# Eight pairs of weights at eight places modulo 512 bytes, and five block bodies that read their columns in five orders

## The reference

```python
# batch 2, sequence 6080, d_model 256, d_ff 2048
sig = 1.0 / (1.0 + np.exp(-f_logit))
f = lower_bound + (1.0 - lower_bound) * sig
i = 1.0 - f
for t in range(S):
    h = f[:, t] * h + i[:, t] * x[:, t]
    y[:, t] = h
...
h = y.reshape(B * S, D) @ w_in                   # 12160 x 256 by 256 x 2048
g = np.where(h > 0.0, h, np.exp(np.minimum(h, 0.0)) - 1.0)
return g @ w_out                                 # 12160 x 2048 by 2048 x 256
```

## Time and profile before

| | |
|---|---|
| median of 2 runs | 963.42 us (961.59 and 965.25) |
| the profiled execution | 962.05 us |
| its span, first to last instruction | 960.2 us |
| TensorE busy | 954.3 us (99%), 4362 matmuls |
| weight loads busy | 815.4 us (85%) |
| ACT, DVE, POOL busy | 790.1, 722.3, 628.8 us |
| granted TensorE clock | 1.000 on average |

### The profile page before, as it was taken

The page is one execution under the profiler, slowest core; times in us unless marked ns, Lnnn a source line. Parts: engine busy times, 40 slices in busy tenths (PEclk is TensorE's granted clock), DMA queues, the critical chain, the costliest instruction groups (busy, mean ns, idle before and its releaser), DMA issues.

```text
span 960.2 us, 15016 instructions
## 1 busy us (share of the span) xinstructions
PE 954.3 (99%) x4362; PEld 815.4 (85%) x4362; DVE 722.3 (75%) x916; ACT 790.1 (82%) x1424; POOL 628.8 (65%) x477
## 2 busy tenths in 40 slices
PE   9999999999999999999999999999999999999998
PEld 6999888888888888888888888888888888888887
DVE  6998876976886796697688679679768867966444
ACT  7989888878888888888888888888888788887775
POOL 2578796576667668557656755856775765676544
PEclk9999999999999999999999999999999999999999
DMA  7212012002101201100210210120021021001001
GB/s 273 68 33 95 0 34 66 34 1 78 55 1 55 77 1 44 55 33 1 75 55 0 66 66 0 45 66 20 23 65 44 0 76 55 0 0 46 1 1 45
DMA packets 23078, 42.02 MB, mean 44 GB/s; under 512 B 2560, under 2 KB 4096, under 8 KB 23040
## 3 DMA queue, kind: packets, MB, share of 16 engines
q1 hardware_dynamic: 22752, 41.10, 13.2%
q10 hardware_dynamic: 288, 0.46, 0.1%
HBM read 29.10 MB, written 12.45 MB: 43 GB/s over the span
## 4 chain that ended last, share of the span: by engine, by line
PE 96%; ACT 2%; DVE 1%; issue 1%; POOL 0%; ACTq 0%; POOLq 0%
PE acc L896 17%; PE acc L898 17%; PE acc L897 17%; PE h L868 14%; PE h L866 14%; PE h L867 14%; ACT e L472 1%; PE h L1010 1%; PE h L1002 1%; PE h L1004 1%; PE h L1003 1%; ACT e L466 1%; DVE x L628 0%; PE h L968 0%; ACT w_out_hi L505 0%
## 5 line engine op out<-in xcount | busy, mean ns | idle before, releaser
L336 POOL TENSOR_TENSOR g_lo<-e,g_hi 128x512 fp32r<-128x512 f32 (+1 forms) x384 | 516.4, 1355 | 325.5 <-ACT g_hi L480 324.0
L466 ACT ACTIVATE e<-h 128x512 f32<-128x512 f32 (+1 forms) x379 | 224.8, 593 | 124.6 <-PE h L868 90.3
L719 DVE SCALAR_TENSOR_TENSOR e<-e,h 128x512 f32<-128x512 f32 (+1 forms) x379 | 256.8, 678 | 70.2 <-ACT e L472 69.1
L896 PE MATMUL acc<-g_hi,w_out_hi 128*128 128x512 f32 (+1 forms) x768 | 291.1, 379 | 0.4 <-DVE w_out_lo L690 0.4
L898 PE MATMUL acc<-g_hi,w_out_lo 128*128 128x512 f32 (+1 forms) x768 | 291.0, 379 | 0.0
L897 PE MATMUL acc<-g_lo,w_out_hi 128*128 128x512 f32 (+1 forms) x768 | 290.9, 379 | 0.0
L472 ACT ACTIVATE e<-e 128x512 f32<-128x512 f32 (+1 forms) x384 | 241.3, 628 | 9.7 <-issue 1.2
L480 ACT CAST g_hi<-e 128x512 fp32r<-128x512 f32 (+1 forms) x384 | 232.1, 604 | 19.3 <-DVE e L719 19.3
L866 PE MATMUL h<-a_hi,w_in_hi 128*128 128x512 f32 x616 | 234.7, 381 | 0.0
L868 PE MATMUL h<-a_hi,w_in_lo 128*128 128x512 f32 x616 | 234.7, 381 | 0.0
L867 PE MATMUL h<-a_lo,w_in_hi 128*128 128x512 f32 x616 | 234.7, 381 | 0.0
(11 more groups left out here) (77 smaller groups left out, 556.0 us busy)
## 6 DMA issues: line engine op xcount, KB each, us to landing
opening<-forget_logit SPq DMA_DIRECT2D x44, 256.0 KB, 2.7
x<-value SPq DMA_DIRECT2D x44, 256.0 KB, 2.7
out<-out_sb SPq DMA_DIRECT2D x44, 256.0 KB, 2.0
w_in_raw<-w_in SPq DMA_DIRECT2D x8, 256.0 KB, 5.4
w_out_raw<-w_out SPq DMA_DIRECT2D x8, 256.0 KB, 6.5
out<-out_sb SPq DMA_DIRECT2D x4, 224.0 KB, 1.9
x<-value SPq DMA_DIRECT2D x3, 224.0 KB, 6.1
opening<-forget_logit SPq DMA_DIRECT2D x2, 224.0 KB, 6.3
```

Source lines behind the costliest of these rows:

```text
L336: nc.gpsimd.tensor_tensor(g_lo[:, t % RING, 0:w], e[:, t % TILES, 0:w], g_hi[:, t % RING, 0:w].bitcast(F32), ALU.subtract).then_inc(g_lo_r ...
L466: nc.scalar.activation(e[:, i, 0:w], bank_of(j, t)[:, 0:w], ACT.Relu, scale=-1.0).then_inc(r_ready, 1)
L719: nc.vector.scalar_tensor_tensor(e[:, t % TILES, 0:w], e[:, t % TILES, 0:w], -1.0, bank_of(j, t)[:, 0:w], ALU.add, ALU.max).then_inc(g_rea ...
L896: nc.tensor.matmul(bank, hi, g_h, start=opens, stop=False)
```

## The change

Two things are changed, and no instruction is added, removed or moved on any engine. Each matmul keeps its place, its weights and its number of columns.

The weights: each pair's row in the four weight tensors is 4 floats (16 bytes, `STEP = 1`) longer. Pair q of `w_in_lo` then lies at q x 16 bytes modulo 512: at 0, 16, 32 to 112. The eight rows of a tensor add 128 bytes to what lies behind it, so that pair q of `w_out_lo` is at 128 + 16 q, of `w_in_hi` at 256 + 16 q and of `w_out_hi` at 384 + 16 q. Modulo 128 bytes (32 columns, the length of a leap in the old order) all four are at 16 q. `out_sb` and the plain `lo` weights of pairs 0 to 3 that block 0 uses (`w_plain_lo`) move to 256 modulo 512. The moving operands stay at multiples of 512: the tensors behind the weights move by 512 bytes in all. `carry`, `slope` and `offset` move into the padding that stood before `opening`.

The orders: `in_order` takes a style (kind, number of groups, columns in a run, direction), and each body gets its own:

| blocks | style | how TensorE steps through 512 columns |
|---|---|---|
| 0 | (T, 4, 8, 0) | as before |
| 1 | (T, 1, 512, 0) | one after the other |
| 2 | (T, 2, 4, 0) | runs of 4, the next one 8 further, 64 times; two groups |
| 3, 5, 7, 9 | (T, 4, 8, 0) | as before |
| 4, 6, 8, 10 | (T, 4, 4, 0) | runs of 4, the next one 16 further, 32 times; four groups |
| 11 | (T, 4, 8, 1) | as before, but the four groups last to first |

```diff
+STEP = 1
...
-LINE = 8
-APART = 4
+T, N = range(2)
+FIRST_STYLE = (T, 4, 8, 0)
+STYLES = (((T, 1, 512, 0),) * 4, ((T, 2, 4, 0),) * 4, ((T, 4, 8, 0),) * 4, ((T, 4, 4, 0),) * 4, ((T, 4, 8, 1),) * 4)
...
-def in_order(columns):
-
-    return columns.rearrange("p (b a c) -> p a b c", a=APART, c=LINE)
+def in_order(columns, style):
+    if style is None:
+        return columns
+    kind, groups, run, down = style
+    if kind == T:
+        steps = columns.rearrange("p (b a c) -> p a b c", a=groups, c=run)
+    elif groups == 1:
+        steps = columns.rearrange("p (o b c) -> p o b c", o=1, c=run)
+    else:
+        steps = columns.rearrange("p (b a c) -> p b a c", a=groups, c=run)
+    if down % 2:
+        steps = steps[:, ::-1]
+    if down // 2 % 2:
+        steps = steps[:, :, ::-1]
+    return steps[:, :, :, ::-1] if down // 4 else steps
...
+        in_row, out_row = in_cols + 4 * STEP, out_cols + 4 * STEP
+
+        def by_product(room):
+            return room[:, :, 0:in_cols].rearrange("p q (k c) -> p q k c", k=PRODUCTS)
...
-        w_in_raw = nc.alloc_sbuf_tensor_at("w_in_raw", [P, PAIRS, PRODUCTS, P], F32, offset=weights_at)
-        w_in_lo = nc.alloc_sbuf_tensor_at("w_in_lo", [P, PAIRS, PRODUCTS, P], F32R, offset=weights_at)
-        w_out_at = weights_at + 4 * PAIRS * in_cols
...
+        w_in_raw = by_product(nc.alloc_sbuf_tensor_at("w_in_raw", [P, PAIRS, in_row], F32, offset=weights_at))
+        w_in_lo = by_product(nc.alloc_sbuf_tensor_at("w_in_lo", [P, PAIRS, in_row], F32R, offset=weights_at))
+        w_out_at = weights_at + 4 * PAIRS * in_row
...
-        w_in_hi = sb("w_in_hi", [P, PAIRS, PRODUCTS, P], F32R)
-        w_out_hi = sb("w_out_hi", [P, PAIRS, 2, D], F32R)
+        w_in_hi = by_product(sb("w_in_hi", [P, PAIRS, in_row], F32R))
+        w_out_hi = by_unit(sb("w_out_hi", [P, PAIRS, out_row], F32R))
...
-        sb("room_of_edge", [P, P - EDGE])
+        edge = sb("edge", [P, P - EDGE])
...
-        carry = sb("carry", [P, BATCH, HALVES, 1])
-        slope = sb("slope", [P, HALVES])
-        offset = sb("offset", [P, HALVES])
+        carry = edge[:, 0:BATCH * HALVES].rearrange("p (b i o) -> p b i o", b=BATCH, o=1)
+        slope = edge[:, 4:4 + HALVES]
+        offset = edge[:, 6:6 + HALVES]
...
-            whole(1, 1)
-            whole(2, 0)
+            whole(1, 1, STYLES[0], FIRST_STYLE)
+            whole(2, 0, STYLES[1], STYLES[0][-1])
             with nc.Fori(1, (BLOCKS - 2) // 2, engines=(mybir.EngineType.PE,),
                          hint_back_edge=True) as i:
-                whole(2 * i + 1, 1)
-                whole(2 * i + 2, 0)
+                whole(2 * i + 1, 1, STYLES[2], STYLES[3][-1])
+                whole(2 * i + 2, 0, STYLES[3], STYLES[2][-1])
             j = BLOCKS - 1
-            whole(j, 1)
+            whole(j, 1, STYLES[4], STYLES[3][-1])
```

More of the change, by code:

```diff
@@ L859, in _, with product @@
         def _(pe):
-            def product(j, par, q, k, bank, start=False):
+            def product(j, par, q, k, bank, style, start=False):
                 w = width(j)
@@ L868, in product, with second @@
                 return nc.tensor.matmul(into, lo, a_h, start=False, stop=True, skip_group_check=True)
-            def second(j, t, half):
+            def second(j, t, half, style):
                 w = width(j)
@@ L902, in second, with whole @@
                     done.then_inc(acc_half, 1)
-            def whole(j, par):
+            def whole(j, par, styles, before):
                 def m(q, back, i, half):
@@ L908, in m @@
                     if at >= 0:
-                        second(j, TILES * at + i, half)
+                        second(j, TILES * at + i, half, styles[q // 2])
                     else:
-                        second(j - 1, TILES * (PAIRS + at) + i, half)
+                        second(j - 1, TILES * (PAIRS + at) + i, half, before)
                 for q in range(PAIRS):
@@ L922, in whole @@
                         pe.wait_ge(g_ready, TILES * (n - 2) + C21 + 1)
-                    product(j, par, q, P1, trunk(q), start=True).then_inc(p1_done, 1)
+                    product(j, par, q, P1, trunk(q), styles[q // 2], start=True).then_inc(p1_done, 1)
                     if q == 0:
@@ L926, in whole @@
                     pe.wait_ge(g_ready, TILES * (n - 1) + C12 + 1)
-                    product(j, par, q, P5, h[:, 2], start=True).then_inc(p5_done, 1)
+                    product(j, par, q, P5, h[:, 2], styles[q // 2], start=True).then_inc(p5_done, 1)
                     m(q, 2, C21, 0)
@@ L967, in first_products @@
                         pe.wait_ge(w_plain_hi_ready, unit // 2 + 1)
[L968 to L969 removed]
+                        nc.tensor.matmul(in_order(first_bank(unit), FIRST_STYLE), plain_weights(unit, half)[0],
+                                         in_order(pieces[half][0], FIRST_STYLE), start=half == 0, stop=False)
                 for unit in range(OPEN):
                     w = TILE if unit < WIDE else SHORT
[L972 removed]
+                    bank = in_order(first_bank(unit)[:, 0:w], FIRST_STYLE)
                     if unit == 0:
                         pe.wait_ge(a_lo_ready[P1], 1)
[L975 removed]
+                    nc.tensor.matmul(bank, plain_weights(unit, 0)[0], in_order(pieces[0][1][:, 0:w], FIRST_STYLE),
                                      start=False, stop=False)
@@ L978, in first_products @@
                     for half in range(HALVES):
-                        nc.tensor.matmul(bank, plain_weights(unit, half)[1], in_order(pieces[half][0][:, 0:w]),
+                        nc.tensor.matmul(bank, plain_weights(unit, half)[1], in_order(pieces[half][0][:, 0:w], FIRST_STYLE),
                                          start=False, stop=False)
@@ L988, in first_product @@
                 b, unit = FIRST_TILES[t]
-                bank = in_order(first_bank(t)[:, 0:SHORT])
+                bank = in_order(first_bank(t)[:, 0:SHORT], FIRST_STYLE)
                 pe.wait_ge(w_plain_lo_ready[unit // 2], 1)
@@ L996, in first_product @@
                     hi, lo = plain_weights(unit, half)
-                    a_h, a_l = [in_order(part[:, 0:SHORT]) for part in a_parts(0, PLACE[b][half])]
+                    a_h, a_l = [in_order(part[:, 0:SHORT], FIRST_STYLE) for part in a_parts(0, PLACE[b][half])]
                     if t == TILES * PAIRS - 2 and half == 0:
-                        nc.tensor.matmul(in_order(h[:, 3]), hi, in_order(a_parts(0, P5)[0]), start=True, stop=False)
+                        nc.tensor.matmul(in_order(h[:, 3], FIRST_STYLE), hi, in_order(a_parts(0, P5)[0], FIRST_STYLE), start=True, stop=False)
                     else:
```

34 lines of the change are left out of this document (18 added, 16 removed).

## The result

The changed kernel takes 1002.33 us (median of 2 runs, 1002.31 and 1002.35) against 963.42. The ratio on record is 1.0413, 95% interval 1.0386 to 1.044 (the two medians alone give 1.0404). It is slower by some 4%. The profiled execution took 1002.35 us, its span is 1000.5 against 960.2: 40.3 us more.

What follows compares the result with a forecast made beforehand. TensorE's single chain of matmuls, 0.220 us a step, was taken as the bound. The profiled 962.05 us plus 11.1 for new orders and 4.1 for shifted weights made 977.2, forecast as 977, range 958 to 1000.

Steps and rivals of the forecast that it cites:

- no term but the step: Whole kernel: no instruction added or moved, so only the time between matmul starts changes; weight loads, DMAs, other engines cost 0.
- Two streams of reads that disturb each other: TensorE: reads of weights and moving columns get in each other's way in some relations and not in others.
- They find a relation without loss after some 14 matmuls.: Block 0 after a pause: step 0.2036 us for fourteen steps, then 0.193; nearly all 3960 later matmuls settled before the change.
- The unsettled price: Each matmul whose two reads have not settled takes 10.3 ns more, read from block 0 after a pause.
- The two terms: Blocks 1 to 11: new orders 11.1 us, shifted weights under the old pattern 4.1 us.
- The new orders: Blocks 1, 2, 4, 6, 8, 10: half of 2160 matmuls unsettled, 11.1 us, bounds 0 and 22.2.
- The shifted weights in the old order: Blocks 3, 5, 7, 9, 11: a quarter of 1575 matmuls unsettled, 4.1 us, bounds 0 and 16.2; pair 0 counted as unmoved.
- Nothing settles: Rival: changes of pair or layer keep upsetting the reads, all 3960 matmuls pay up to 10.3 ns, about 1003 us; chance 0.12.
- the four signs: Wrong if step 0.220 everywhere, follows order but not pair, is below 0.220 for long, or TensorE waits on another engine.
- leaps: Rival: the order's 64 runs cost 3.3 ns a matmul; block 1 gains 1.2 us, blocks 2 to 10 even lose 5.9; chance 0.10.

Runs made afterwards that it cites:

- the run at 128: Kernel before, old order, all weights 128 bytes further and moving operands still at multiples of 512: 1001.3 to 1001.7 us.
- the run at 16: Kernel before, old order, all weights at 16 modulo 512 and moving operands at 32: 1008.2 to 1008.7 us.

## Why the prediction was wrong

The range was 958 to 1000 and the time is 1002.33. The direction was right, the size was not.

**What bounds the kernel, and no term but the step.** Right. TensorE is the only bound, before and after: it is busy for 99% of both spans, and after the change its only waits are of 1.6 and 1.3 us. The prediction's 2.4 GHz can be read from the steps at a granted clock of 1.000: 512 columns take 220.0 ns and 448 take 193.3, so 64 columns take 26.7 and one 0.417, which is 2.4 columns in a nanosecond.

**Two streams of reads that disturb each other.** Supported, as far as the step can show it. The relative place of weights and moving operand decides (both moved by 32 bytes: no change; weights alone by 128: 229.5; other distances: 226.7 to 236.7), the order of the reads decides (226.7 in plain order), and the order of the writes doesn't (220.0 either way). As the prediction said, the step changes by pair in the old order too (227.4 to 234.2 in block 5). It had pair 0 of those blocks at 220, and it is at 227 to 228. No run names the unit in which they meet, so the collision itself remains an inference.

**"They find a relation without loss after some 14 matmuls."** This is the step that failed. I took it from block 0, where it is true of 448 columns at place 0 after one pause (the rows left out there are thirteen, not eleven; the fourteen steps are right). The same trace has four pauses in block 0. Behind those that end at 45.9 and 52.5 us the step is 0.193 from the third matmul on, and the one at 49.8 is followed by the next before it settles. So the fourteen come from a single pause. The rows behind the pause at 52.5:

```profile
52.46 0.44 PE L1002 MATMUL h<-a_hi,w_in_hi 128*128 128x448 f32 x1
52.74 0.36 PE L1003 MATMUL h<-a_lo,w_in_hi 128*128 128x448 f32 x1
52.94 0.35 PE L1004 MATMUL h<-a_hi,w_plain_lo 128*128 128x448 f32 x1
53.13 0.35 PE L1002 MATMUL h<-a_hi,w_in_hi 128*128 128x448 f32 x1
53.33 0.35 PE L1003 MATMUL h<-a_lo,w_in_hi 128*128 128x448 f32 x1
53.52 0.35 PE L1004 MATMUL h<-a_hi,w_plain_lo 128*128 128x448 f32 x1
```

A chain of 512 columns wasn't seen to do so. For the old order at the old places it had one of two steps, 220.0 or 230.7, and it stayed at 230.7 for the rest of the kernel: for 3240 matmuls in the run with one plain block, and by their times (37 us more) in four executions with one split matmul. The unsettled price was thus not one of 14 matmuls but of all.

**The two terms.** The new orders were put at half of 22.2 us, 11.1; they cost 4.4 + 4.4 + 4 x 2.4 = 18.4. Their upper bound held for the sum, but blocks 1 and 2 were 12 ns over before, against its 10.3. The shifted weights in the old order were put at a quarter of 16.2 us, 4.1; they cost 4 x 3.7 + 5.0 = 20. Here the bound failed too, on two counts: the price is up to 13.9 ns in block 11 where the rows gave 10.3, and pair 0 isn't spared; the run at 128 shows that 128 bytes are no period. The remaining 1.9 us, in block 0 and behind block 11, were put at nothing.

**The rival "Nothing settles".** It gave 1003 and was nearest, and I gave it 0.12. That the number fits so well is luck in part: it had 10.3 ns in every block, and the blocks paid from 6.7 (4 x 4) to 13.9 (block 11). Its reason was too narrow as well. It blamed the changes between weights at different places, but weights at one common other place cost as much (229.5 ns at 128), and so does one block in another order (230.7). What I held against it, that changes between layers occur every 6 to 9 matmuls and cost nothing, was badly weighed: all those weights lay at the same place modulo 512, so by my reading nothing had changed for the two streams. None of the four signs that I named for being wrong came about, so they didn't watch the step of the reasoning that failed. Of "leaps", the run with plain output and the one with plain order refute the price: fewer leaps made 220 into 226.7, and none on the output made no difference.

**The weights' place alone, and leaps on the output.** Moving the weights alone by 128 bytes costs 39.5 us of 962 with the same instructions on TensorE, whose only waits in that trace are one of 1.3 us and one of 0.9. The output's 64 runs of 8 columns cost nothing: 961.84 us with them, 961.79 with a contiguous output.

**What stays open.** Whether the changed kernel's places have no step of 220 or whether only the change from pair to pair loses it. For the first speaks that the distances of -16, 16 and 128 never showed it in four executions each; for the second that 48 did, once, and that the changed kernel has stretches of four to nine steps at 220, most of which end where the weights' place changes. The run with half of the pairs moved doesn't decide it, since none of its pairs had the old distance. What makes the length of a cycle isn't known either. What loses the state in the kernel before (by their times five of 42 executions from early on, two in the last block; none of these was traced) was seen in the trace of the run moved by 32 bytes, some 12 us behind the loop's end, and its cause wasn't tried.

## What to carry to other kernels

Where TensorE's chain is dense, read the step from start to start and not the busy share: TensorE was busy 99% of the span at a step of 220 and at one of 230. Look for the step's pattern too. Here 219, 221 over and over was one state of the chain and 230, 230, 237, 228, 229 another, and the same kernel had the first by its times in 35 of 42 executions. One common place for all weights wasn't enough: of five distances modulo 512 bytes between weights and moving operands, only that of 0 gave the 962 of a 220 step in most executions, in the old order. Suspect every odd-sized matmul, change of order or padding: here one matmul split in two went with 37 us more, by the times of four executions, one block in plain order with 41, and weights 128 bytes further with 39.5, each on 962. Work out the address of the moving operands too when you shift the weights: three of the shifts here moved both. A test of an access pattern inside one kernel can measure the state that it inherits as well: the old order had 230.7 behind one plain block and 220.0 without it. To measure the pattern, run a kernel that has it throughout, several times.

## What the runs showed that I had not expected

- The step has memory. Identical instructions at identical places took 220.0 or 230.7 ns each for some 750 us, by what came before.
- The shortest steady step seen in a long fp32r chain is 220.0 for 512 columns and 193.3 for 448, both 6.7 ns over the columns at the 0.417 ns each that the difference of the two gives, and it was seen in an order with leaps. The plain order had 226.7.
- The cycles repeat to within a nanosecond: 240, 232, 222 over and over in the run at 16; 230, 230, 237, 228, 229 in the old order at distance 0 once 220 is lost. Two times at least, and so two states, were seen at distance 0 (962 and 1004.5 us), at 48 (962 and 988) and, for runs of 4, at 64 (988 and 1008).
- The two odd values of the kernel before fit with it: 1004.5 is 962 and eleven blocks at 10.7 ns more for each matmul (42.4 us), and 965.6 in the run moved by 32 bytes is 962 and the 334 matmuls behind the loss in its trace (3.6 us). The 965.2 of the kernel before would be some 300 matmuls.
